# Moving one unit's normalisation behind the first two chunks' scaling on VectorE and ScalarE

## What is computed

```python
mag = sqrt(a_re*a_re + a_im*a_im)
scale = minimum(mag, 0.999) / (mag + 1e-6)
a = (a_re*scale, a_im*scale)              # complex decay per token and channel
for t in range(768):                      # batch 4, heads 8, head size 48
    S = a[t] * S + outer(k[t], v[t])      # S complex, 48 x 48 per head
    y[t] = q[t] @ real(S)
x = max(x@w1, x@w2, x@w3) @ w_out         # 3072 tokens, 384 -> 768 -> 384
# then: 8 experts, 384 -> 1024 -> 384, one per token, weighted by its gate
```

## Time and profile before

| | |
|---|---|
| median of 3 runs | 894.49 us (893.66 to 896.08) |
| profiled execution, its own time | 893.84 us |
| its span | 892.1 us |
| busy share PE, DVE, ACT, POOL | 88%, 73%, 56%, 54% |
| mean granted clock of TensorE | 0.966 of full speed |

### The profile page before, as it was taken

One profiled execution on the slowest core, in us unless ns is written; L12 is line 12 of the kernel. 1 busy time (PEld: TensorE's weight loads), 2 busy tenths in 40 slices (PEclk: granted clock), 3 DMA queues, 4 the chain that ended last, 5 costly groups with the idle time before them and its releaser, 6 DMA issues.

```text
span 892.1 us, 18729 instructions
## 1 busy us (share of the span) xinstructions
PE 786.7 (88%) x6641; PEld 728.5 (82%) x6642; DVE 649.4 (73%) x1051; ACT 497.7 (56%) x1033; POOL 478.7 (54%) x768
## 2 busy tenths in 40 slices
PE   0568897789989999999999999919999999999995
PEld 0436797788879898988999999918999999997894
DVE  5989899799999999999897755288323353558821
ACT  5696966676868777777566563234211242437511
POOL 1199999899979797979765000013223233333222
PEclk9769999999999999999999999968999999999998
DMA  9401152452424252423321110445511141417211
GB/s 310 132 11 43 50 148 83 95 154 77 119 76 113 77 130 81 119 73 82 95 71 43 42 42 30 153 170 172 190 35 62 46 168 64 171 48 283 83 36 45
DMA packets 41875, 89.73 MB, mean 101 GB/s; under 512 B 6264, under 2 KB 23680, under 8 KB 40480
## 3 DMA queue, kind: packets, MB, share of 16 engines
q1 hardware_dynamic: 37632, 76.04, 28.3%
q0 software_dynamic: 4160, 12.60, 4.4%
HBM read 69.74 MB, written 17.69 MB: 98 GB/s over the span
## 4 chain that ended last, share of the span: by engine, by line
PE 51%; DVE 21%; issue 9%; POOL 9%; ACT 7%; DMA 2%; SPq 0%; ACTq 0%; DVEq 0%; POOLq 0%
PE yu L1799 4%; PE yu L1803 4%; PE yu L1800 4%; PE mm L1799 3%; PE mm L1800 3%; PE mm L1803 3%; POOL c_re L2179 2%; PE tr L2081 2%; PE mm L2083 2%; PE mm L2081 2%; PE mm L2082 2%; PE tr L2082 2%; PE tr L2083 2%; DVE l_im L1222 2%; DVE h_sb L1241 2%
## 5 line engine op out<-in xcount | busy, mean ns | idle before, releaser
L1799 PE MATMUL mm<-up_hi,x_hi 128*128 128x384 f32 x432 | 156.4, 362 | 12.3 <-DVE h_sb L1241 9.1
L2179 POOL TENSOR_TENSOR c_re<-ring 112x128 f32<-112x128 f32 x165 | 126.5, 766 | 51.4 <-DVE ring L1194 37.3
L1800 PE MATMUL mm<-up_lo,x_hi 128*128 128x384 f32 x432 | 146.6, 339 | 0.0
L2264 POOL DMA_INDIRECT out_rows<-g_o,rows_out x30 | 35.2, 1175 | 143.9 <-DVE g_o L1634 135.2
L1799 PEld LDWEIGHTS mm<-up_hi,x_hi 128*128 128x128 f32 x432 | 81.7, 189 | 21.1 <-DVE h_sb L1241 12.4
L1803 PE MATMUL mm<-up_hi,x_lo 128*128 128x384 f32 x432 | 98.7, 336 | 0.0
L2183 POOL TENSOR_TENSOR c_im<-turn,ring 112x128 f32<-112x128 f32 x105 | 73.9, 704 | 28.9 <-ACT turn L738 28.7
L2240 POOL DMA_INDIRECT g_in<-x_scratch,rows_in x34 | 37.5, 1102 | 92.0 <-DVE rows_in L1602 66.9
L1799 PE MATMUL yu<-e_hi,gh_hi 128*128 128x384 f32 x240 | 82.2, 342 | 0.0
L1800 PEld LDWEIGHTS mm<-up_lo,x_hi 128*128 128x128 f32 x432 | 81.9, 190 | 0.0
L1800 PE MATMUL yu<-e_lo,gh_hi 128*128 128x384 f32 x240 | 80.7, 336 | 0.0
(11 more groups left out here) (268 smaller groups left out, 2336.3 us busy)
## 6 DMA issues: line engine op xcount, KB each, us to landing
raw<-in_moe_w SPq DMA_DIRECT2D x16, 1536.0 KB
a_dn<-in_a_laid SPq DMA_DIRECT2D x18, 384.0 KB, 6.7
an_scratch<-a_dn SPq DMA_DIRECT2D x18, 384.0 KB, 2.3
ring<-an_scratch SPq DMA_DIRECT2D x18, 384.0 KB, 5.7
q_in<-in_q_laid SPq DMA_DIRECT2D x24, 224.0 KB, 2.8
k_in<-in_k_laid SPq DMA_DIRECT2D x24, 224.0 KB, 3.1
v_in<-in_v_laid SPq DMA_DIRECT2D x24, 192.0 KB, 3.3
x_scratch<-x_sb SPq DMA_DIRECT2D x24, 192.0 KB, 2.6
```

Of the source, the lines that this page charges most:

```text
L1799: nc.tensor.matmul(out, hi[:, x, :], w_hi(x), start=(x == 0), stop=False)
L1800: nc.tensor.matmul(out, hi[:, x, :], w_lo(x), start=False, stop=False)
L2179: nc.gpsimd.tensor_tensor(c_re[:, 0:count, :, :], cur, bc(prev[:, :, 0, :], 2, 2), ALU.mult).then_inc(chain_prod, 1)
```

## The change

On ScalarE `norm_square(5)` and `norm_mag(5)` go behind the steps of chunk 0 that stood after them, `norm_rsqrt(5)` goes from the start of round 0 behind `z_recip(1)`, `norm_rest(5)` goes behind `y_copy(0)`, ahead of the low copies 16 to 20, and `z_square(1)` goes ahead of `norm_rest(4)`. On VectorE `norm_m2(5)` goes behind `z_norm(0)`, `norm_sum(5)` behind `k_decay(0)`, `norm_inverse(5)` behind `k_decay(1)`, and `norm_apply(4)` between `z_norm(1)` and `add_state(0)`. No instruction is added or removed; TensorE, GpSimd and SyncE keep their lists.

```diff
 # ScalarE, head
-            norm_square(5, norm_of(5))
             norm_mag(4, norm_of(4))
             stage_z(0)
             z_square(0)
-            norm_mag(5, norm_of(5))
+            norm_square(5, norm_of(5))
             z_recip(0)
             low_copy(range(8, 12))
+            norm_mag(5, norm_of(5))
 # ScalarE, rounds
                 if n == 0:
                     norm_rsqrt(4, norm_of(4))
-                    norm_rsqrt(5, norm_of(5))
...
+                if more and not late_z:
+                    z_square(n + 1)
                 if n == 0:
                     norm_rest(4, norm_of(4))
-                if more and not late_z:
-                    z_square(n + 1)
...
                 if n == 0:
-                    norm_rest(5, norm_of(5))
                     low_copy(range(12, 14))
...
                 if more:
                     z_recip(n + 1)
+                if n == 0:
+                    norm_rsqrt(5, norm_of(5))
...
                     y_copy(0)
+                    norm_rest(5, norm_of(5))
                     low_copy(range(16, LOWS - KF + 3))
 # VectorE, head
-            norm_m2(5, norm_of(5))
             norm_sum(4, norm_of(4))
             z_norm(0)
-            norm_sum(5, norm_of(5))
+            norm_m2(5, norm_of(5))
             z_newton(0)
             q_decay(0)
             k_decay(0)
+            norm_sum(5, norm_of(5))
 # VectorE, rounds
                 if n == 0:
                     norm_inverse(4, norm_of(4))
-                    norm_inverse(5, norm_of(5))
-                    norm_apply(4, norm_of(4))
...
                     z_norm(n + 1)
+                if n == 0:
+                    norm_apply(4, norm_of(4))
                 if now:
                     add_state(n)
...
                     k_decay(n + 1)
                 if n == 0:
+                    norm_inverse(5, norm_of(5))
                     norm_apply(5, norm_of(5))
```

## The result

The changed kernel takes 898.17 us (median of 11 runs), the kernel before beside it 894.23: a ratio of 1.0045, 95% interval 1.0034 to 1.0057. In two later groups of runs, on the same chip as the kernels tested there, the ratio was 1.0037 (1.0023 to 1.0051) and 1.0047 (1.0029 to 1.0066). By the first interval it is slower by 3 to 5 us, by the two later ones by 2 to 6. The time lies in the predicted range and on the side of rival (a), not of the case that I had called likeliest (896.4).

A forecast was written before the change was run, and what follows sets the result against it. The chain runs through VectorE and ScalarE, unit nine's store and load, then GpSimd. Lateness of 1.4 + 0.7 = 2.1 us, 0.9 kept, gives 893.84 + 1.9 = 895.7, plus 0.65 for the median: 896.4 us; range 892.5 to 898.7.

The forecast's parts named there:

- rival (a): TensorE's clock stays at 1.2 GHz through blocks 18 to 22 and more; 897.5 to 898.5 us; chance 0.28.
- the case that I had called likeliest: VectorE's round 1 goes late, 1.9 us reach the end, 896.4 us; chance 0.40.
- The lead in the head: ScalarE's and VectorE's start of chunk 0, without unit five's square ahead: z_newton(0) 0.52 us earlier, at 61.06.
- Round 0 on VectorE: k_decay(1) ends 2.3 us earlier, but norm_apply(5) waits for norm_rest(5); net gain nothing, bounds minus 0.8 to plus 0.4.
- What is late next: ScalarE's low copies 16 to 20 start 2.5 us late behind norm_rest(5); 1.4 us of lateness reach VectorE at chunk 2.
- The clock: TensorE's 3.3 us wait may drop it to 1.2 GHz; between nothing and some 3 us, taken as 0.7.
- What survives: Of 2.1 us late at chunk 2 on VectorE, 0.9 of it, 1.9 us, reaches unit nine's store and the end.
- (b): Late low copies are absorbed by VectorE's small waits around 94 to 163 us or shorter GpSimd steps; 894 to 895.2; chance 0.18.
- (c): VectorE's lead, 0.5 to 0.8 us, reaches the norms of units six to nine; 892.5 to 893.8; chance 0.14.
- the inner part of (c): The smaller gains from VectorE's lead, those that the range from 892.5 us takes in.
- the class with 0.60: The outcome "the same", no change beyond 0.3%, between 891.8 and 897.2 us; chance 0.60.

The follow-up runs named there:

- experiments 1: Changed kernel with norm_rest(5) moved behind low copies 16 to 20 on ScalarE: 896.2 us, ratio 1.0005 to the kernel before; again 894.84 us, 0.9997.
- Experiment 6: Changed kernel with norm_inverse(5) between z_newton(1) and q_decay(1) on VectorE: 894.16 us, ratio 0.9988 to the kernel before; again 894.6 us, 0.9995.
- experiment 2: Changed kernel with TensorE computing low block 17 five times instead of once: 895.8 us, ratio 1.0003 to the kernel before; again 894.9 us, 1.0000.
- experiment 3: Changed kernel with unit five's norm_rsqrt, norm_inverse and norm_rest back in their old places: 895.63 us, ratio 1.0002 to the kernel before.
- experiment 5: Kernel before with only norm_apply(4) moved between z_norm(1) and add_state(0) on VectorE: 894.85 us, ratio 1.0000.
- experiment 4: Kernel before with only norm_inverse(5) and norm_rest(5) late: 900.56 us, ratio 1.0060; second, also with block 17 computed seven times: 897.72 us, 1.0036.

## Why the prediction went as it did

**The lead in the head** (0.52 us at `z_newton(0)`): 61.58 to 61.11, so 0.47. Right.

**Round 0 on VectorE.** `k_decay(1)` was to end at 78.10 and ended at 76.93 + 1.36 = 78.29; the inverse at 79.78, it ended at 79.75; `norm_rest(5)` at 80.55, it ended at 80.50; `norm_apply(5)` at 82.54, it ended at 82.49, and `join(1, 0)` began at 82.70. Right: the earlier decays are paid back by the wait for `norm_rest(5)`, 0.79 us, and the gain on VectorE is nothing.

**What is late next.** The low copies from 80.55: from 80.41. Right, and the chain that ended last runs through it; experiments 1 and 6, which each move one step, remove the stall and the loss with it.

**The clock** was the step that failed. The prediction put it as "I take one block's worth, 0.7". It measured 2.46 us up to copy 23 in this execution, and 1.63 to 2.90 over the three, by experiment 2. So scores(1) came at 86.19 and not at 83.5, where experiment 2, with the clock up, had them at 83.98. The hole was 3.98 us and not 3.3, because TensorE had answers(0) and blocks 16 and 17 at the higher clock and finished them by 77, and in all three profiled executions of the changed kernel the clock fell in it or, once, 0.1 us behind it. The Trainium skill, "TensorE: Matmul & The Clock Gate", section "HAM oscillation — how this bites in real kernels", warns of such gaps between matmuls, and the falls at the holes of 3.98, 4.11 and 4.61 us agree with it. I had set one wait of 2.59 us without a fall against it, which was a shorter one.

**What survives.** "Some of it dies on the way to unit nine's store at 153.49, in small waits for other engines; I keep 0.9 of it, 1.9 us." So 2.1 us late at `z_norm(2)` were to be 1.9 at unit nine and at the end. In the changed kernel 4.26 us at `z_norm(2)` were 4.5 at unit nine, whose application had started at 152.50, and 3.6 at the end of the profiled execution. The wait at 163 grew to 2.89 us, a little short of the 3 that I had named.

How much dies between 98 and 153 us goes with the clock in that stretch, and not with how late `z_norm(2)` is. In the executions without a fall between 102 and 165 us some dies: 3.80 us became 2.68 and 2.06 (98.23 against 96.17) became 0.92 in the two of experiment 2, 3.12 became 2.64 in experiment 3, and 0.54 became -0.59 in experiment 5. In those with one or two falls nothing or next to nothing does: 3.70 became 4.18, 4.78 became 4.84 and 4.26 became 4.50 in the three of the changed kernel, 7.13 became 7.62 in the first of experiment 4, and 0.6 to 0.9 us stayed 0.5 to 1.0 in the four of experiments 1 and 6. The first of these falls in the changed kernel lies on the chain that ended last, where the same matmul takes 0.33 us and later 0.17:

```profile
111.28 0.33 PE yu L1843
...
115.87 0.17 PE yu L1843
```

So the later falls go with up to one and a half us more at unit nine, by comparison of single executions of different kernels; no run tests them alone. The prediction had no term for them. Whether the filled hole is what spared experiment 2 these later falls, or only where they happened to lie in two executions, stays open, and with it how the 3.9 us at the end divide. That some 1 us at unit nine need not show in the time, experiments 1, 2 and 6 say: unit nine is 0.5 to 1.0 us late in five of their profiled executions, and their medians cannot be told from that of the kernel before.

**The rivals.** (a) was right: "scores(1) and copy 23 are 4 to 5.5 us late" (4.9 and 4.9), 897.5 to 898.5 (898.17), though the lower clock lasted through blocks 18 to 20 only and not on to 22. It had 0.28. (b), the absorbed stall, is what the time looks like if the clock is held up, experiment 2. One thing that it had named did happen in the changed kernel: GpSimd's steps ran shorter, so that it was through with group 2 at 120.77 and not at 124.49. It gained nothing, since it then waited for the load of group 3. (c) wanted `k_decay(1)` and the inverse done before 78.5. Experiment 6 makes only the inverse so early (77.3); `k_decay(1)` ended at 81.03. The stall is gone, yet no lead of VectorE is left at round 1, which began 0.7 to 0.9 us later than before. The medians are 0.8 and 0.0 us under the kernel before and the intervals reach down to 2.1 us, so the inner part of (c) is neither shown nor excluded. In experiment 5, where `norm_apply(5)` did end early, the join waited 1.02 us for GpSimd. That wait stood in no part of the prediction.

**The chances.** The range held because it took in all of (a); the likeliest case missed by 1.8 us, and the class with 0.60, no change beyond 0.3%, is not what came. Of 0.32 for slower, 0.28 were on the right mechanism. With a hole longer than both waits that I had compared it to, the fall should have been the main case and not the rival.

## What to carry to other kernels

When a step is moved behind others, look at both queues: on the engine that waits, list what stands behind the waiting instruction, and follow that to the engine that it feeds. The decays were 2.2 us earlier and nobody could use them, because copies that had nothing to do with them stood behind the new wait. And if the engine at the end of that list is TensorE, price the hole by its clock first. Here a stall of 2.9 to 3.6 us with the clock held up cost nothing that could be measured; with the fall, half of the 3.4 to 6.1 us at the lower level was lost at once, and 3.8 us at the end. Look also at what the moved work meets next: decays that are ready early are of no use if the join behind them then waits for GpSimd.

## What the hardware showed unexpectedly

Five copies of a low block's matmuls instead of one, pure waste, made the changed kernel faster by 3.8 us in the same group. In its three profiled executions a hole of 3.98 to 4.61 us came with a fall of the clock each time, and the clock stayed at 0.50 through 3.4 to 6.1 us of full work, in which a pair of these matmuls took 1.51 us instead of 0.82. With the hole filled up to 1.23 us or less there was none. Shorter waits went either way: the kernel before had a fall at 72.9, 1.6 us behind its wait of 1.75 us at 71.32, the changed kernel none behind one of 1.80 us at 70.91.

GpSimd waited 5.51 us at 126.28 for the load of group 3, a wait that the kernel before does not have. It had come there 3.7 us earlier than before and went on 1.6 us later; the chain that ended last was on TensorE then and does not run through the wait.
